# Attention and two feed-forward layers on one core: the first batch's queries and keys pooled on TensorE instead of VectorE

## What is computed

```python
q_d = q.reshape(B, H, Sd, 4, D).mean(axis=3)      # 576 tokens -> 144, keys and values alike
out_d = sm_attn(q_d, k_d, v_d)                    # softmax(q_d k_d^T / 8) v_d
mask = np.abs(pos[:, None] - pos[None, :]) < 4
out_local = softmax(where(mask, q k^T / 8, -1e9)) v
x = repeat(out_d, 4) + out_local                  # -> 2304 x 512
h = x @ w_in;  x = (h * clip(h + 3, 0, 6) / 6) @ w_out      # d_ff 2048
out = max(x @ w1, x @ w2, x @ w3) @ w_out2                  # d_ff 768
```

## Time and profile before

| | |
|---|---|
| median of 3 runs | 787.93 us (787.21 to 788.32) |
| the profiled execution | 787.94 us, span 786.1 us |
| mean granted TensorE clock | 0.997 of full speed |
| TensorE busy | 770.9 us, 98% of the span |
| VectorE busy | 413.7 us, 53% |
| ScalarE busy | 299.6 us, 38% |
| GpSimd busy | 221.7 us, 28% |

### The profile page before, as it was taken

The page is one execution under the profiler, slowest core; times in us unless marked ns, Lnnn a source line. Parts: engine busy times, 40 slices in busy tenths (PEclk is TensorE's granted clock), DMA queues, the critical chain, the costliest instruction groups (busy, mean ns, idle before and its releaser), DMA issues.

```text
span 786.1 us, 13594 instructions
## 1 busy us (share of the span) xinstructions
PE 770.9 (98%) x5398; PEld 668.3 (85%) x5398; DVE 413.7 (53%) x786; ACT 299.6 (38%) x671; POOL 221.7 (28%) x280
## 2 busy tenths in 40 slices
PE   7889999999999999999999999999999999999998
PEld 6667777878888787888888889999988999899996
DVE  5865465356355445535445553646681555625650
ACT  4746555344343444334344453522241211412221
POOL 7855756321122022111227760013200111011110
PEclk9999999999999999999999999999999999999999
DMA  9992422122211221210418877797203660137302
GB/s 182 200 262 63 129 62 63 33 85 63 62 24 40 64 86 31 63 33 2 156 48 299 298 277 273 255 345 256 95 16 132 244 238 1 54 121 252 123 1 81
DMA packets 95435, 100.50 MB, mean 128 GB/s; under 512 B 61580, under 2 KB 79500, under 8 KB 95372
## 3 DMA queue, kind: packets, MB, share of 16 engines
q1 hardware_dynamic: 92692, 98.74, 39.3%
q10 hardware_dynamic: 2680, 0.89, 0.6%
HBM read 73.66 MB, written 25.95 MB: 127 GB/s over the span
## 4 chain that ended last, share of the span: by engine, by line
PE 90%; DVE 3%; POOL 2%; ACT 2%; DMA 1%; issue 1%; SPq 1%; ACTq 0%; DVEq 0%; POOLq 0%
PE bank L846 28%; PE bank L848 27%; PE bank L847 27%; PE bank L981 1%; PE bank L958 1%; PE bank L903 1%; PE bank L947 1%; PE bank L920 1%; DMA k_nat_c<-in_k_dram 1%; PE bank L933 1%; POOL w L760 1%; PE bank L865 1%; POOL dp_a L752 1%; PE bank L875 1%; DMA b_raw<-in_moe_w_dram 0%
## 5 line engine op out<-in xcount | busy, mean ns | idle before, releaser
L1600 DVE SCALAR_TENSOR_TENSOR rg<-rg,bank 128x512 f32<-128x512 f32 (+1 forms) x80 | 50.7, 634 | 150.4 <-ACT rg L1273 150.4
L846 PE MATMUL bank<-xo,wt 128*128 128x384 f32 x378 | 126.4, 334 | 1.2 <-ACT p L1405 1.2
L848 PE MATMUL bank<-xo,wt 128*128 128x384 f32 x378 | 126.3, 334 | 0.0
L847 PE MATMUL bank<-xo,wt 128*128 128x384 f32 x378 | 126.3, 334 | 0.0
L846 PE MATMUL bank<-xs,w 128*128 128x512 f32 (+1 forms) x320 | 121.6, 380 | 1.6 <-DVE xs L1572 0.9
L846 PE MATMUL bank<-gs,w 128*128 128x512 f32 (+1 forms) x320 | 121.7, 380 | 0.1
L848 PE MATMUL bank<-xs,w 128*128 128x512 f32 (+1 forms) x320 | 118.3, 370 | 0.0
L847 PE MATMUL bank<-xs,w 128*128 128x512 f32 (+1 forms) x320 | 118.1, 369 | 0.0
L847 PE MATMUL bank<-gs,w 128*128 128x512 f32 (+1 forms) x320 | 118.1, 369 | 0.0
L848 PE MATMUL bank<-gs,w 128*128 128x512 f32 (+1 forms) x320 | 117.9, 369 | 0.0
L1273 ACT ACTIVATE rg<-bank,half 128x512 f32<-128x512 f32 (+1 forms) x80 | 51.4, 643 | 144.2 <-PE bank L848 144.2
(11 more groups left out here) (246 smaller groups left out, 1199.8 us busy)
## 6 DMA issues: line engine op xcount, KB each, us to landing
wt<-t_scratch SPq DMA_DIRECT2D x19, 1792.0 KB, 7.8
t_scratch<-ph SPq DMA_DIRECT2D x9, 896.0 KB, 3.6
t_scratch<-pl SPq DMA_DIRECT2D x9, 896.0 KB, 6.6
b_raw<-in_moe_w_dram SPq DMA_DIRECT2D x9, 512.0 KB, 3.8
xr<-x_scratch SPq DMA_DIRECT2D x3, 1536.0 KB, 7.1
out_dram<-o_sb SPq DMA_DIRECT2D x18, 256.0 KB, 2.0
w_raw<-in_moe_w_in_dram SPq DMA_DIRECT2D x16, 256.0 KB, 3.9
w_raw<-in_moe_w_out_dram SPq DMA_DIRECT2D x16, 256.0 KB, 4.9
```

The lines of the kernel that those rows point to most:

```text
L846: mm(dst, w[0], m[0], start=start, stop=False, skip_group_check=True)
L847: mm(dst, w[0], m[1], start=False, stop=False, skip_group_check=True)
L848: return mm(dst, w[1], m[0], start=False, stop=stop, skip_group_check=True)
L1600: vec.scalar_tensor_tensor(out=gated(s), in0=gated(s), scalar=1.0, in1=hidden_bank(s)[:, 0:n], op0=ALU.min, op1=ALU.mult).then_inc(s_g, 1)
```

## The change

For pairs 0 to 3 the pooled queries and keys are no longer summed by VectorE from `qT` and `kT`. GpSimd writes a matrix `groups` (128 x 24, ones where row // 4 equals the column) after the identity and before the masks. Right after the last two transposes of `turn_k(n)`, TensorE multiplies each of the pair's twelve landed 96x128 blocks with it: the block is the stationary operand, the 96x24 matrix the moving one, in fp32, and the result (features x 24 groups) goes beside the last two key blocks in the bank `bc`, 2 x 144 columns. The semaphore that tells ScalarE of the last key blocks is raised only after that. ScalarE copies the two halves to `qd` and `kd` in `copy_pooled(n)`, queued right behind `copy_k(n)`. For the narrow pairs 1 and 2, `scores_local` also waits for these copies. Pairs 4 to 15 stay as they are.

```diff
--- before.py
+++ after.py
@@ -297,6 +297,8 @@
         maskb = work("maskb", [P, 2, TPH, KW], BF16)
         identb = work("identb", [P, P], BF16)
 
+        groups = work("groups", [P, RQ // FACTOR])
+
         mask_raw = work_c.lp
 
         STEP0, STEP1 = bank[2], bank[1]
@@ -391,6 +393,7 @@
         s_tqk = sem("s_tqk")
         s_cqk = sem("s_cqk")
         s_pool = sem("s_pool")
+        s_groups = sem("s_groups")
         s_sl = sem("s_sl")
         s_madd = sem("s_madd")
         s_lmax = sem("s_lmax")
@@ -693,6 +696,12 @@
             g.affine_select(out=ident[:], in_=ident[:], compare_op=ALU.not_equal, fill=1.0, base=0,
                             pattern=[[-1, P]], channel_multiplier=1).then_inc(s_ident, 1)
 
+            chain(g.memset(groups[:], 1.0))
+            chain(g.affine_select(out=groups[:], in_=groups[:], compare_op=ALU.is_ge, fill=0.0, base=0,
+                                  pattern=[[-FACTOR, RQ // FACTOR]], channel_multiplier=1))
+            g.affine_select(out=groups[:], in_=groups[:], compare_op=ALU.is_ge, fill=0.0, base=FACTOR - 1,
+                            pattern=[[FACTOR, RQ // FACTOR]], channel_multiplier=-1).then_inc(s_groups, 1)
+
             def lay_mask(m, edge_of, done):
 
 
@@ -866,6 +875,18 @@
                 mine.then_inc(s_tqk, 1)
                 turn(t.bb[:, 0:RQ], to.q[:, 5, :], ident[0:RQ, 0:RQ])
 
+            def pooled(n):
+
+                to, t = land(n), tiles(n)
+
+                pe.wait_ge(s_groups, 1)
+                for i, src in enumerate((to.q, to.k)):
+                    for j in range(J):
+                        a = 2 * RQ + i * SD + j * RQ // FACTOR
+                        mine = mm(t.bc[:, a:a + RQ // FACTOR], src[:, j, :], groups[0:RQ], start=True, stop=True,
+                                  skip_group_check=True)
+                return mine
+
             def turn_k(n):
                 to, t = land(n), tiles(n)
                 turn = nc.tensor.transpose
@@ -879,12 +900,17 @@
                     pe.wait_ge(s_cqk, 4 * n + 1)
                 for j in range(4, 6):
                     mine = turn(t.bc[:, (j - 4) * RQ:(j - 3) * RQ], to.k[:, j, :], ident[0:RQ, 0:RQ])
+                if n < PAIRS:
+                    mine = pooled(n)
                 mine.then_inc(s_tqk, 1)
 
             def scores_local(n):
                 t = tiles(n)
 
                 pe.wait_ge(s_cqk, 4 * n + 4)
+                if narrow(n):
+
+                    pe.wait_ge(s_pool, 2 * n + 2)
                 if n < PAIRS:
 
                     pe.wait_ge(s_mb, 1)
@@ -1190,6 +1216,13 @@
                 act.wait_ge(s_tqk, 3 * n + 3)
                 fn(to_k[:, 4 * RQ:S], t.bc[:, 0:2 * RQ], ACT.Copy).then_inc(s_cqk, 1)
 
+            def copy_pooled(n):
+                t = tiles(n)
+
+                act.wait_ge(s_tqk, 3 * n + 3)
+                fn(t.qd[:], t.bc[:, 2 * RQ:2 * RQ + SD], ACT.Copy, scale=SCALE).then_inc(s_pool, 1)
+                fn(t.kd[:], t.bc[:, 2 * RQ + SD:2 * RQ + 2 * SD], ACT.Copy).then_inc(s_pool, 1)
+
             def exp_local(n):
                 t = tiles(n)
 
@@ -1342,11 +1375,14 @@
             fn(maskb[:], mask_raw[:], ACT.Copy).then_inc(s_mb, 1)
             copy_q(0)
             copy_k(0)
+            copy_pooled(0)
             copy_q(1)
             copy_k(1)
+            copy_pooled(1)
             copy_q(2)
             exp_local(0)
             copy_k(2)
+            copy_pooled(2)
             exp_down(0)
             copy_local(0)
             copy_turned(0)
@@ -1358,6 +1394,7 @@
             copy_q(3)
             copy_local(1)
             copy_k(3)
+            copy_pooled(3)
             copy_turned(1)
             exp_down(2)
             copy_down(1)
@@ -1671,16 +1708,13 @@
             dve.wait_ge(s_ident, 1)
             vec.tensor_copy(identb[:], ident[:]).then_inc(s_idb, 1)
             dve.wait_ge(s_zero, 1)
-            pool_qk(0)
             max_masked(0)
             sub_masked(0)
-            pool_qk(1)
             max_down(0)
             inverse_local(0)
             max_masked(1)
             inverse_down(0)
             sub_masked(1)
-            pool_qk(2)
             max_masked(2)
             max_down(1)
             sub_masked(2)
@@ -1690,7 +1724,6 @@
             inverse_local(2)
             split_low(0, 0, 0)
             max_down(2)
-            pool_qk(3)
             max_masked(3)
             inverse_down(2)
             sub_masked(3)
```

## The result

The changed kernel takes 800.57 us, median of four runs (798.97 to 803.74), against 788.12 for the kernel before in the same comparison (787.21 to 788.98): a ratio of 1.0171 with a 95% interval of 1.0156 to 1.0187. It is slower, by somewhat less than 2%. The forecast was 794.3 with a range up to 797.5. The profiled execution took 800.26 us with a span of 798.5, so +12.3 against the 787.94 of the kernel before.

A forecast was written before the change was run, and what follows sets the result against it. The prediction took TensorE, busy for 98% of the span, to bound the kernel. The path sum 4P - 4.08 with P = 2.6 gave +6.3 us on 787.94, so 794.3 us, range 789.0 to 797.5.

The forecast's parts named there:

- P: TensorE's time for one pair's pooled(n): 24 weight loads at 0.108 us, so 2.6 us.
- Leg 1: pooled(0) starts at 8.63; the last key copy waits for it, so scores_local(0) starts at 9.26 + P.
- Leg 2: pooled(1) starts at 10.60 + P; scores_local(1) waits 0.98 for pooled copies; scores_down(0) shifts by 3P - 1.04.
- Leg 3: From scores_down(0) to turn_q(3) the chain keeps its lengths, so the shift stays the same.
- Leg 4: pooled(3) and its two copies delay copy_turned(1) and exp_down(2) behind it; exp_down(2) moves by 4P - 1.12.
- Leg 5: norm_down(2) had waited behind sum_v(3)'s transfer; that slack takes 2.08 us off the shift, leaving 4P - 3.20.
- the clock falls during pooled(n): Rival: TensorE drops to half clock in pooled blocks; two pairs so cost +5.2 us, about 799.5; chance 0.08.
- A granted clock under 1 before 30: Sign that the forecast is wrong: TensorE's granted clock below full before 30 us in the profile after.
- 4P - 3.20: Forecast shift of norm_down(2), low_w1(0) and hidden(0) after the transfer's slack, before any gain from the clock.
- leg 6: No idle stretch before turn_down(2), so hidden(0)'s first six products run at full clock: 1.33 instead of 2.21, -0.88 us.
- Carried to the end one for one: After hidden(0) TensorE is nearly always busy, so the shift there reaches the kernel's end unchanged.
- The removal is worth nothing: Taking eight reduces (0.74 us each) off VectorE gains nothing on the path, being covered by TensorE and GpSimd.

The follow-up runs named there:

- experiment 3: Changed kernel with one idle bf16 product of 128x256 ahead of each pooled product; 796.33 us, ratio 1.0121.
- experiment 11: Changed kernel with pair 0 left to VectorE and pooled products of pairs 1 to 3 moved to where idle products stood; 798.22 us, ratio 1.0138.
- experiment 12: experiment 11 with one idle bf16 product of 128x256 ahead of each pooled product; 789.28 us, ratio 1.0023.
- experiment 2: Changed kernel with 56 instead of 24 columns in each pooled product, the additional ones unused; 796.87 us, ratio 1.0124.
- experiment 1: The changed kernel run again without alteration, beside its variants on one chip; 799.98 us, ratio 1.0158.
- experiment 4: Kernel before with 24 idle bf16 products where each pooled block would stand, nothing else of the change; 794.64 us, ratio 1.0103.
- experiment 5: Kernel before with VectorE's eight pooling reduces of pairs 0 to 3 cut to one group each; 787.58 us against 787.63, ratio 0.9999.
- experiment 8: Changed kernel with only pairs 0 and 1 pooled by TensorE, the others by VectorE as before; 791.19 us in one run.

## Why the prediction was wrong

The direction was right and half of the size was missing: +6.3 forecast, +12.3 measured. By the prediction's own steps:

- **P, the deciding term, was right**: 2.62 for three of the pairs, by 24 x 0.109, forecast 2.6 by 0.108. The choice of the slope of the other loads over that of the transposes is borne out. The rule of the Trainium skill beside it ("TensorE: Matmul & The Clock Gate", LDWEIGHTS) gives 107 ns, and the trace's spacing of 109 agrees, though a load's own duration in the profile is 192; at half clock the spacing is 208, where that rule has no clock in it.
- **Legs 1 to 5 were right in what waits for what.** Leg 1: pooled(0) starts at 8.63. Leg 2: pooled(1) should start at 10.60 + P = 13.22 and did at 13.27, and scores_local(1) waits its 0.98 (16.89; 16.82 by the leg). Leg 3: max_down(0) +10.56, turn_q(3) +10.55. Leg 4: exp_down(2) 41.06, +13.02, by the leg 10.55 + 2.62 - 0.08 = 13.09. Leg 5: norm_down(2) +10.69, so 2.33 fell away where 2.08 was forecast.
- **The failed step is the clock**, the rival "the clock falls during pooled(n)", given only 0.08, while every leg of the main case took full clock for granted. A granted clock under 1 before 30 was named there as a sign of being wrong, and it is 0.50 from 17.5 on. By the legs scores_down(0) should be 3P - 1.04 = 6.8 late; it is 10.03. Of the 3.2, pooled(2) has 2.5 (5.13 instead of 2.62) and scores_local(1) and turn_k(2) before it 0.7. Scores_down(0) itself takes 0.5 longer. The second fall makes keep_warm(12) end after low_w1(0), 0.6 later at hidden(0). Together that is 4.3; legs 4 and 5 came out 0.3 cheaper than forecast, so that in all hidden(0) is 11.27 late, 4.0 more than 4P - 3.20 = 7.28. The argument that I gave against the rival, 1.00 through all transposes and scores, was a row of a stretch that held no block of pooled products; it could not speak for them. The rival's price, 799.5, came out close to 800.6, but not by its own sum: it had two pairs at half clock (+5.2), where one pair ran so (+2.5), and the rest came from the scores and transposes beside it, from the wait of leg 6 below and from the second fall; that the sums meet is luck. Experiments 3, 11 and 12 show the cause: with an idle product ahead of each pooled one the fall doesn't come, and the kernel is faster for more work. Experiment 2 adds that it comes later with more columns between the same loads.
- **Leg 6 failed too.** It took 0.88 off since the first six products of hidden(0) would run at full clock. They did (0.23 from start to start), but turn_local(3) came 2.98 after hidden(0) began, not 1.33: the second half waits 0.77 for split_low, which VectorE reaches only behind pair 3's inverse_local, and turn_local(3) waits 0.30 for norm_local(3). In place of -0.88 it is +0.77. In experiments 1, 3 and 4, where the clock is full here, the distance is 2.46 to 2.47, in the kernel before 2.21. So even at full clock leg 6 would be +0.25, since what the products save is lost in waits; the other 0.52 goes with the second fall, under which values_local(1) came later, so that VectorE's put_x(1) waited 1.76 for it instead of the 0.67 of these three. What is waited for is pair 3's softmax. Scores_local(3) stands behind pooled(3) and starts 12.80 late (40.17, before 27.37), with no wait for a transfer to hide a part of it, where low_w1(0) is 10.69 late. Before, GpSimd went from low_w1(0) to norm_local(3) without waiting (36.42); here it waits 1.83 for linv_a, and in experiments 1, 3 and 4 0.73 to 0.74.
- **Carried to the end one for one: nearly.** turn_local(3) is 12.04 late, the end of the span 12.4. From the second step on the shift is 11.73 (57.47, before 45.73), and it grows by 0.69 at one wait of TensorE for VectorE, which stands behind ScalarE's work on a weight block (b_raw) whose transfer lets ScalarE start 12.42 later (475.39, before 462.97). The row of before, then of after:
```profile
466.91 0.39 PE L846 MATMUL bank<-xs,w 128*128 128x256 f32 x1 [0.41 <-DVE rg L1600]
```
```profile
479.33 0.39 PE L855 MATMUL bank<-xs,w 128*128 128x256 f32 x1 [1.10 <-DVE rg L1637]
```
Why this transfer is later by more than the products around it isn't shown.
- **The removal is worth nothing**, as forecast (experiment 5). The groups' building moved the mask by 0.7 at most, behind the pooled products, as forecast.

The sum as measured: 7.28 for the path less 0.3 in legs 4 and 5, 4.8 for the clock (4.3 up to hidden(0) and 0.5 behind it), 0.25 for leg 6 at full clock, 0.3 later: 12.3. Forecast: 7.2, 0 for the clock, -0.88 for leg 6, 0 later.

In experiment 4 the medians differ by 7.5 and the starts of hidden(0) by 5.3. Of these 2.2, 1.3 lie between the executions (the two profiled ones differ by 6.2 only, the opening being shorter), and 0.9 in the trace behind hidden(0): 0.25 up to turn_local(3), most of the rest at the same late wait as above. In experiment 8 it is 1.5, of which 1.15 lie in the trace; I haven't followed them.

What stays open: why the clock falls in these blocks (that idle products between them prevent it is shown, by what is not), what brought the fall that is left in experiment 2, and why the second fall comes in some executions and not in others.

## What to carry to other kernels

A block of small fp32 products with full-width weights cost its loads here, not its columns, and before such a block is put on the path its effect on the clock has to be priced beside its length: here 2.6 us a block on the path, and up to twice that once the clock had fallen. Idle products that stand in a tuned order may be what holds the clock up: whoever replaces them by real work should look at the granted clock afterwards, before judging the place. One idle bf16 product ahead of each fp32 product, that is one for every two loads, cost 0.37 us a block and kept the clock. And a slot in which an engine waits anyway took the same work for under a third of the price: 0.66 us a pair on average over three pairs in experiment 12, where it also took the place of 26 idle products, and 2.3 over four in experiment 3.

## What the runs showed of the hardware

TensorE's clock fell to 1.2 GHz without an idle stretch ahead of it: from 8 to 17.5 PE waited for 0.30 us in all, its busy share was 4.00 of 4.00 at 8 to 12 and at 12 to 16, that of the loads 3.88 and 3.93, and at 17.5 the granted clock went to 0.50. The Trainium skill ("TensorE: Matmul & The Clock Gate", Part 1) says that the clock is gated by how busy the array has lately been; the trace agrees only if that means something else than the profile's busy share, which gave no warning here. At the low clock the spacing of the pooled records doubled nearly (208 against 109 ns), while a load's own duration went only from 192 to 333 ns.

The granted clock of the first microseconds is not to be read from the table: it gives 1.00 for 0 to 34 in the earlier trace rows, while the 30 idle products at the opening take 6.28 us, 0.20 each, and 24 of the same take 2.6, 0.109 each, in experiment 4.

A bf16 128x256 product slipped in between two fp32 products with 128-column loads cost 0.03 us (0.249 against 0.218 for the group), where a row of such products alone is spaced by 0.109 (experiment 4: 24 in 2.6 us).
